# Low passes of gate and value for the last 64 features as a pair of row tiles in units 6 to 76

## What is computed

```python
def _moe_ref(x, w_gate, w_val, w_out, rms_g):
    rms = np.sqrt(np.mean(x * x, axis=-1, keepdims=True) + 1e-06)
    xn = x / rms * rms_g
    g = xn @ w_gate                       # 320 -> 1536
    silu = g * (1.0 / (1.0 + np.exp(-g)))
    val = xn @ w_val                      # 320 -> 1536
    return (silu * val @ w_out)           # 1536 -> 320

def _moe2_ref(x, w_gate, w_val, w_out):
    gate = 1.0 / (1.0 + np.exp(-(x @ w_gate)))
    val = x @ w_val
    return (gate * val @ w_out)
```

## Time and profile before

| | us |
|---|---|
| median of 3 runs | 466.35 (466.12 to 466.36) |
| the profiled execution | 466.2 |
| its span, first to last instruction | 464.1 |
| TensorE busy | 457.6 (99%), 3067 matmuls |
| VectorE busy | 222.6 (48%) |
| ScalarE busy | 186.5 (40%) |
| GpSimd busy | 34.1 (7%) |

### The profile page before, as it was taken

One profiled execution on the slowest core, in us unless ns is written; L12 is line 12 of the kernel. 1 busy time (PEld: TensorE's weight loads), 2 busy tenths in 40 slices (PEclk: granted clock), 3 DMA queues, 4 the chain that ended last, 5 costly groups with the idle time before them and its releaser, 6 DMA issues.

```text
span 464.1 us, 7889 instructions
## 1 busy us (share of the span) xinstructions
PE 457.6 (99%) x3067; PEld 377.7 (81%) x3067; DVE 222.6 (48%) x436; ACT 186.5 (40%) x385; POOL 34.1 (7%) x69
## 2 busy tenths in 40 slices
PE   8999999999999999999999999999999999999997
PEld 4699998788788787888888888888888888888885
DVE  6779668776565364555544552222322222322223
ACT  7866456544543241465444552222322222322222
POOL 4264111111010000000000000000000000000000
PEclk9999999999999999999999999999999999999999
DMA  7673046520220200003233200000100000100001
GB/s 211 199 235 105 23 146 196 163 73 16 60 59 25 101 2 1 1 1 96 96 101 111 65 0 0 1 1 1 50 6 1 0 1 0 57 1 0 1 0 57
DMA packets 15836, 26.29 MB, mean 57 GB/s; under 512 B 2264, under 2 KB 10808, under 8 KB 15800
## 3 DMA queue, kind: packets, MB, share of 16 engines
q1 hardware_dynamic: 15576, 25.68, 18.3%
q10 hardware_dynamic: 224, 0.12, 0.1%
HBM read 23.55 MB, written 1.97 MB: 55 GB/s over the span
## 4 chain that ended last, share of the span: by engine, by line
PE 94%; DVE 3%; ACT 1%; issue 1%; DMA 1%; DVEq 0%; ACTq 0%
PE bank L1520 54%; PE bank L1612 8%; PE bank L1614 7%; PE bank L1613 7%; PE bank L1620 3%; PE bank L1621 3%; PE pair L1460 2%; PE pair L1437 2%; PE bank L1559 1%; PE pair L1474 1%; PE pair L1426 1%; PE bank L1393 1%; PE bank L1492 1%; PE bank L1507 1%; DMA fi_row<-fi_first 1%
## 5 line engine op out<-in xcount | busy, mean ns | idle before, releaser
L1520 PE MATMUL bank<-x_hi,gv_split 128*128 128x512 f32 (+1 forms) x770 | 234.6, 375 | 0.6 <-issue 0.6
L1520 PEld LDWEIGHTS bank<-x_hi,gv_split 128*128 128x128 f32 x770 | 141.6, 188 | 26.8 <-issue 0.9
L1520 PE MATMUL bank<-x_lo,gv_split 128*128 128x512 f32 (+1 forms) x430 | 159.9, 374 | 0.0
L1185 DVE TENSOR_TENSOR hid<-hid,bank 128x512 f32<-128x512 f32 x48 | 33.0, 687 | 132.4 <-PE bank L1520 132.4
L692 ACT ACTIVATE hid_hi<-hid 128x512 fp32r<-128x512 f32 (+1 forms) x78 | 46.7, 598 | 121.1 <-DVE hid L1185 90.5
L1520 PEld LDWEIGHTS bank<-x_lo,gv_split 128*128 128x128 f32 x430 | 80.9, 188 | 14.1
L685 ACT ACTIVATE hid<-bank 128x512 f32<-128x512 f32 (+1 forms) x78 | 43.9, 563 | 119.3 <-PE bank L1520 88.6
L1192 DVE TENSOR_TENSOR hid_lo<-hid,hid_hi 128x512 fp32r<-128x512 f32 (+1 forms) x78 | 51.6, 661 | 40.2 <-ACT hid_hi L692 40.2
L1612 PE MATMUL bank<-hid_hi,wo_split 128*128 128x512 f32 (+1 forms) x154 | 59.9, 389 | 0.2 <-DVE hid_lo L1192 0.2
L1614 PE MATMUL bank<-hid_hi,wo_split 128*128 128x512 f32 (+1 forms) x154 | 57.5, 373 | 0.0
L1613 PE MATMUL bank<-hid_lo,wo_split 128*128 128x512 f32 (+1 forms) x154 | 57.4, 373 | 0.0
(11 more groups left out here) (204 smaller groups left out, 377.2 us busy)
## 6 DMA issues: line engine op xcount, KB each, us to landing
gv_raw<-wgv SPq DMA_DIRECT2D x24, 384.0 KB, 3.2
qk_tile<-qk SPq DMA_DIRECT2D x24, 160.0 KB
wo_raw<-wo SPq DMA_DIRECT2D x24, 160.0 KB, 3.6
v_sb<-v SPq DMA_DIRECT2D x12, 168.0 KB, 4.6
gate<-og SPq DMA_DIRECT2D x12, 160.0 KB, 2.7
k_sb<-k SPq DMA_DIRECT2D x10, 160.0 KB, 4.7
outT<-y_out SPq DMA_DIRECT2D x6, 256.0 KB, 2.0
rhs<-log_split SPq DMA_DIRECT2D x16, 4.0 KB
```

Source lines behind the costliest of these rows:

```text
L1185: ins = nc.vector.tensor_tensor(h, h, v_ps[:, 0:size], ALU.mult)
L1520: mm = pe.matmul(ps[:, 0:size], lhs, rhs, start=(i == 0), stop=whole and i == len(passes) - 1)
```

## The change

A new function `paired(u)` is true in units 6 to 76. It takes the place of `has_group(u)` in the three functions and calls below; `has_group` stays where it orders the work of ScalarE and VectorE. So 55 more units leave out the two eighth passes and issue `tail_products`: 6, 7, 8, 17, 22, 25 and 28 to 76.

```diff
+def paired(u):
+
+    return SPLIT <= u < UNITS - 1
...
-                mm = hidden(g_ps, 0, f, start, size, not has_group(u))
-                if not has_group(u):
+                mm = hidden(g_ps, 0, f, start, size, not paired(u))
+                if not paired(u):
                     mm.then_inc(g_done, 1)
...
-                mm = hidden(v_ps, 1, f, start, size, not has_group(u))
-                if not has_group(u):
+                mm = hidden(v_ps, 1, f, start, size, not paired(u))
+                if not paired(u):
                     mm.then_inc(v_done, 1)
...
-                if has_group(u):
+                if paired(u):
                     tail_products(u)
```

## The result

The changed kernel takes 478.21 us (478.12 to 479.03, 5 runs) against 466.35 (466.12 to 466.8, 5 runs): 1.026 times as long, 95% interval 1.0247 to 1.0269. It is slower by 11.9 us; 11.2 to 11.4 were forecast. The profiled execution has a span of 476.3 us, 12.2 more than before.

A forecast was written before the change was run, and what follows sets the result against it. The prediction took TensorE to be the bound, from matmul start to start. It added 8.5 + 0.5 + 0.8 + 0.9 + 0.7 = 11.4 us to 466.2, giving 477.6 us, range 472 to 481.

The forecast's parts named there:

- Bound by TensorE, start to start: Whole kernel: TensorE busy 99% of the span; the distance between matmul starts counts, 0.227 us a pass of 512 columns.
- In 0.32, out 0.43, second output pass 0.335: Late units: steps around the pair total 1.085 us against 0.907 for four passes, so 0.178 us slower a unit.
- 0.43 over 0.34: Step from pair to first output pass: 0.43 us taken; rivals with 0.34: 466 (load hidden, chance 0.04), 472 (exposed, 0.08).
- Units 29 to 76: 48 late units at 0.178 us each, 8.5 us, all on the path as TensorE has no gap there.
- the slow passes (item 5): First full passes after each return run slightly slow: 0.015 us a unit, 0.7 us; rival 0.06 a unit, 479.8, chance 0.12.
- Units 6 to 8 and 17 to 28: Early new units: 0.8 us in units 6 to 8, 0.5 in units 17, 22, 25, 28, and 0.9 of stalls.
- the two stalls: TensorE held back by VectorE: 0.4 us around units 6 to 8, 0.5 us at unit 18, together 0.9 us.
- The late gate result: Gate results come later: covered in late blocks, 0.9 us of stalls in early units; rival that it bounds: 482, chance 0.04.
- The rival with the whole pass saved: All new units: tiles enter without a stop and each pair saves a whole pass; -12.2 us, so 454, chance 0.05.

The follow-up runs named there:

- deferred_full: Kernel before, but in the 55 new units the two eighth passes stay full 128-row passes and stand behind the value passes, where the pair would; 467.51 us.
- late_only: Kernel before with pairs added in units 29 to 76 only; units 6, 7, 8, 17, 22, 25 and 28 as before; 476.12 us.
- three_pairs: As the kernel with pairs added in units 29 to 76 only, plus two more pairs behind the pair in units 31 to 76, into unread banks; 497.26 us.
- batch_two: Kernel before, with units 30 to 75 taken two at a time, both pairs back to back, then output passes of the two units before; 468.52 us.
- same_rows: Changed kernel, but in the 55 new units both tiles of the pair stand on rows 64 to 127; 492.05 us.
- the control: Kernel before plus, in units 31 to 76, one extra 64-column matmul of 128 rows into an unused bank, ahead of the output passes; 472.76 us.
- switch_only: Kernel before plus, in units 31 to 76, one extra 64-column matmul of 64 rows into an unused bank, ahead of the output passes; 486.02 us.

## Why the prediction was right

By its own steps:

1. *Bound by TensorE, start to start*: right. Late units show no wait, and what each step costs is what the time grows by.
2. *In 0.32, out 0.43, second output pass 0.335*: all three as read (0.32, 0.43 and 0.34 in the late unit above), with no row of the exact step out to go by. The choice of 0.43 over 0.34 carried the forecast; the return to 128 rows costs what the change to another small shape did. The drain on a change of mode that TensorEngine Tiling (Array Packing) of the Trainium skill states under Key Properties agrees with it: each change of shape costs 0.09 us, and 0.11 more for a load that isn't hidden. That the 0.09 is the draining itself no row shows; the rows show only that it comes with the change of shape.
3. *Units 29 to 76*: 9.76 us against 8.5 + 0.7. The term that was too small is the slow passes (item 5). I halved it, as a pair is only two instructions; in 46 late units of the trace it is 0.023 on average, and the three steps are 0.180 us longer than four passes, where I had 0.178. Together that is 0.203 a unit; the forecast had 0.193. 48 x 0.01 is the 0.5 us by which it fell short.
4. *Units 6 to 8 and 17 to 28*: 2.16 us against 2.2, the two stalls where they were expected.
5. *The late gate result*: no wait in blocks 2 to 5, the end of block 2 included, and 1.2 us in units 7, 8 and 18 by deferred_full, where the forecast had 0.9: right in place and nearly in size.
6. 0.23 us of the span came before anything was changed, in the first units; it isn't a part of any step. The same stretch is 0.05 longer in late_only and 0.29 in deferred_full, so it varies from trace to trace.

The rival with the whole pass saved, from the up to 2x of TensorEngine Tiling (Array Packing) of the Trainium skill (section Theoretical Speedup), isn't wrong of the tiles: three_pairs shows the factor for a pair behind a pair. It leaves out the way in and out.

What the reading got wrong without harm is what the 0.43 is made of. I took it for a pass and 0.20 for leaving the shape; 0.11 of that 0.20 is the load of the pair's own weights, which the first matmul of a shape pays and the next ones don't. With 0.43 as the way out behind any number of pairs, batch_two had to lose 2 us by the shapes; they cost it nothing, and it lost 2 us by waits.

## What to carry to other kernels

A pair of small tiles between full passes must save more than its round trip, here 0.43 us or 1.9 passes of 512 columns: one pair saves a pass and so loses 0.2 us net, two come out even, and by three_pairs a third would earn 0.23. So look for neighbours of the same shape first, and read the price from the step from start to start on either side of a shape change, not from the matmul's own duration or from how many rows of the array it fills. When the price of a step rests on one row, ask which part of it the first of a kind pays alone; an experiment that adds a second of the kind shows it.

## What the runs showed of the hardware that was not expected

- The weight load of the first matmul of a tile shape is exposed (0.11 us), in either direction; in the changed kernel the loader is idle for 0.35 us ahead of the pair and for 0.24 ahead of the first output pass. The load of the second is hidden, even on the same rows (same_rows: 0.34 to the second tile, then 0.33 out).
- After the return from a pair of 512 columns, and also after the control's 64-column matmul without any change of shape, some five passes run at 0.228 to 0.236 instead of 0.227. In the control the two rows behind 391.18 are 391.41 and 391.65; in switch_only, with one small matmul of 64 rows, they are at 0.227 again. What causes it isn't settled.
